# Three stages on one core: matmul order between heads, and attention and first layer in one block

## The chip, the cores and the metric

The kernel runs on one core of a Trainium2 chip. The metric is the time of one execution in microseconds (us); lower is better. The engines are named PE (TensorE, matmuls), ACT (ScalarE), DVE (VectorE), POOL (GpSimd) and SP (SyncE, which issues nearly all transfers here). Each engine runs its own list of instructions in order, and they wait for each other by semaphores.

## The reference

Three stages follow each other. Attention over 2 x 8 heads with 768 tokens of 64 numbers, masked by a hash: a score counts only where the signs of six projections of q and of k agree.

```python
mask = q_bucket[:, :, :, None] == k_bucket[:, :, None, :]
scores = np.where(mask, scale * (q @ k.T), -1e9)
scores -= max(scores); attn = exp(scores); attn /= sum(attn) + 1e-9
x = attn @ v                          # 1536 tokens x 512
h = np.maximum(x @ w_in, 0.0)         # first layer, 512 -> 2048
y = h * h @ w_out                     # 2048 -> 512
# experts: 8 experts of capacity 192, tokens assigned greedily by sorted logits y @ w_gate
out[mask_e] = np.maximum(y[mask_e] @ w1[e], 0.0) @ w2[e]
```

## The kernel before

**Attention (lines 74 to 681).** Sixteen heads are taken in the order of `ORDER`, in pairs: an even and an odd head. Pairs 1 to 6 run in a hardware loop on PE and on DVE; pair 0 and the last heads are written out. For a head n the parts are: `scores` (six steps of 128 queries, one matmul pass) from which DVE takes row maxima (`row_max`, `max_done`); `rows`, which turns the maxima and a sum of v into rows by small matmuls; ACT copies these rows (`qb`, line 317, `v_sum_hi`, line 318) and DVE makes `v_low`; `scores_t`, the transposed scores with the maximum folded in, six steps; ACT takes the exponential of each (`expo`, line 324, into `pt`); `fallback` and `weighted` multiply by v and accumulate in PSUM. Each `weighted` is one half of a step and shows as two records, as its operands are plain fp32. `scores` of head n+1 are mixed into head n on PE. There is one PSUM slot of two banks for the transposed scores, so `scores_t` j+1 waits for `expo` j.

During an even head the next pair is prepared: `t_k` and `t_q` transpose k and q, ACT copies the high parts (`k_high`, `q_high`, line 313), DVE subtracts for the low parts (`k_low`, `q_low`, line 391), `z_k` and `z_q` project them (lines 512 to 514), and DVE makes the bits (`k_bits`, `q_bits`). SP copies the parts from there into the operands of each head (`assemble`, lines 168 to 181): it first waits until all `scores_t` of the head two before are through, then issues eight copies; `q_high` of the next pair waits until those of the odd head have landed (lines 306 to 313).

When a head is through, DVE copies the numerator (line 426) and ACT the denominator (line 330); DVE takes reciprocals in four quarters (`invert`, line 432), POOL divides (`divide`, line 271), ACT and POOL split the quotient into `xt_hi` and `xt_lo` (`high`, line 335; `low`, line 277). The weights of the first layer are loaded by SP during the heads, in 17 transfers counted by `w_ready`.

**First layer (lines 706 to 1049).** A block of its own; a block ends when all engines have reached its end. Four chunks of 384 tokens by 16 tiles of 128 hidden units. For a tile g ACT makes `wi_hi` and `wo_hi` (lines 829, 836) and POOL `wi_lo` and `wo_lo` (lines 750, 756), in two buffers each. PE runs `hidden` (12 matmuls, line 965) into one of two banks, ACT relu and square (lines 842, 844), DVE the product `h` and the difference `h_lo` (lines 889, 892), and PE `rows` (9 matmuls, line 976) of the tile, one tile behind. The first chunk also finishes the last head: DVE takes reciprocals of two halves ahead of its tiles 0 and 1 (lines 907, 910), POOL divides after `both_low` of tile 0 (line 780), ACT and POOL split after tiles 2 and 3.

**Experts (lines 1052 to 1437).** Routing on DVE and PE in small steps, then eight experts, with gathers and scatters by POOL. DVE starts with a memset of the tail of `slot_onehot` (line 1331); POOL waits for the stores of y ahead of its first gather.

## Time and profile before

| | |
|---|---|
| median of 3 runs | 879.3 us (878.26 to 882.99) |
| the profiled execution's own time | 880.77 us |
| its span, first to last instruction | 879.0 us |
| mean granted TensorE clock | 0.961 |
| PE busy | 815.8 us, 93% |
| DVE, ACT, POOL busy | 411.1, 321.6, 281.6 us |

Attention takes the span up to 312.5 us, the first layer from there to about 610 us, routing and experts the rest. The page gives the span in 40 slices of 22 us. In a timeline each line is one or several like instructions in order of time; "idle" in brackets is how long the engine had nothing to run before it, and who released it. A PE record starts when its operands begin to be read, and records overlap: the distance between two starts is the pace.

### The profile page before, as it was taken

What the parts mean: (1) busy time and instruction counts of PE and PEld (TensorE: products, weight loads), DVE (VectorE), ACT (ScalarE), POOL (GpSimd) and SP (SyncE); (2) the same over time, 40 slices, a digit from 0 to 9 for tenths busy, and PEclk for the clock granted to TensorE, in tenths of its full rate; (3) what the DMA queues carried; (4) which work ended last, traced back from release to release, by engine and by line L of the source; (5) the groups of instructions that cost most, each with busy time, mean ns of one, the idle gap of its engine ahead of it and who ended that gap; (6) DMA issues with size and microseconds to landing.
All of it is one profiled execution on the core that took longest, in us unless ns stands there. A gap on an engine that the chain in (4) does not pass through costs nothing. (4 is left out here: it accounts for less than half of the span.)

```text
span 879.0 us, 13881 instructions
## 1 busy us (share of the span) xinstructions
PE 815.8 (93%) x4688; PEld 698.8 (79%) x4688; DVE 411.1 (47%) x884; ACT 321.6 (37%) x575; POOL 281.6 (32%) x283
## 2 busy tenths in 40 slices
PE   5999999999999969999999999997389998999996
PEld 3767777677776758999999999996279998999996
DVE  7466666666666545224223223423634554455410
ACT  1344434444344444554554555452011212112211
POOL 3022322223222246655665566562000101110101
PEclk8799999999999989999999999999579999999999
DMA  7345545567635300001000001000235453635351
GB/s 166 71 104 122 126 101 126 131 143 176 143 90 137 93 0 1 0 0 37 0 0 36 0 0 37 0 0 37 97 114 210 144 199 118 224 131 209 141 201 36
DMA packets 65763, 81.28 MB, mean 92 GB/s; under 512 B 41304, under 2 KB 41304, under 8 KB 65216
## 3 DMA queue, kind: packets, MB, share of 16 engines
q1 hardware_dynamic: 63680, 74.54, 30.8%
q0 software_dynamic: 2048, 6.29, 2.2%
q8 instruction: 20, 0.33, 0.1%
q14 instruction: 15, 0.12, 0.0%
HBM read 54.55 MB, written 6.29 MB: 69 GB/s over the span
## 5 line engine op out<-in xcount | busy, mean ns | idle before, releaser
L586 PE MATMUL banks<-pt,v_raw 128*128 128x384 f32 x384 | 149.3, 489 | 0.0
L324 ACT ACTIVATE pt<-banks 128x768 f32<-128x768 f32 x96 | 78.0, 812 | 137.5 <-PE banks L536 135.5
L889 DVE TENSOR_TENSOR h<-relu 128x384 f32<-128x384 f32 x64 | 42.1, 658 | 177.3 <-ACT relu L842 177.2
L750 POOL TENSOR_TENSOR wi_lo<-w_in_sb,wi_hi 128x512 fp32r<-128x512 f32 x64 | 84.0, 1313 | 95.3 <-ACT wi_hi L829 94.3
L403 DVE TENSOR_REDUCE mx<-banks 128x1 f32<-128x768 f32 x96 | 89.9, 951 | 30.3 <-PE banks L563 28.5
L1405 PE MATMUL banks<-x_cols,w_in_sb 128*128 128x192 f32 x512 | 96.1, 340 | 1.3 <-ACT x_cols L1189 1.1
L1419 PE MATMUL banks<-expert_hidden,w_out_sb 128*128 128x192 f32 x512 | 93.4, 333 | 0.0
L965 PE MATMUL banks<-xt_hi,wi_hi 128*128 128x384 f32 (+1 forms) x256 | 87.5, 342 | 6.2 <-POOL wi_lo L750 6.2
L756 POOL TENSOR_TENSOR wo_lo<-w_out_sb,wo_hi 128x512 fp32r<-128x512 f32 x64 | 83.8, 1309 | 15.0 <-ACT wo_hi L836 15.0
L1405 PEld LDWEIGHTS banks<-x_cols,w_in_sb 128*128 128x128 f32 x512 | 84.5, 195 | 3.7 <-issue 2.0
L965 PE MATMUL banks<-xt_lo,wi_hi 128*128 128x384 f32 (+1 forms) x256 | 87.0, 340 | 0.0
L965 PE MATMUL banks<-xt_hi,wi_lo 128*128 128x384 f32 (+1 forms) x256 | 86.8, 339 | 0.0
L1419 PEld LDWEIGHTS banks<-expert_hidden,w_out_sb 128*128 128x128 f32 x512 | 83.1, 192 | 0.8
L586 PEld LDWEIGHTS banks<-pt,v_raw 128*128 128x128 f32 x384 | 68.9, 189 | 15.3 <-issue 3.3
L535 PE MATMUL banks<-qa,ka 128*128 128x384 f32 x192 | 72.1, 376 | 8.0 <-ACT pt L324 4.7
L976 PE MATMUL banks<-wo_hi,h_hi 128*128 128x512 f32 x192 | 76.2, 397 | 2.2 <-DVE h_lo L892 2.1
L563 PE MATMUL banks<-kb,qb 128*128 128x384 f32 x192 | 74.5, 472 | 2.4 <-DVE qb L399 2.1
L976 PE MATMUL banks<-wo_hi,h_lo 128*128 128x512 f32 x192 | 76.3, 397 | 0.0
L976 PE MATMUL banks<-wo_lo,h_hi 128*128 128x512 f32 x192 | 76.0, 396 | 0.0
L536 PE MATMUL banks<-qb,kb 128*128 128x384 f32 x192 | 65.2, 339 | 0.0
L842 ACT ACTIVATE relu<-banks 128x384 f32<-128x384 f32 x64 | 31.5, 493 | 91.5 <-PE banks L965 91.5
L535 PEld LDWEIGHTS banks<-qa,ka 128*128 128x128 f32 x192 | 36.5, 190 | 29.3 <-ACT pt L324 15.1
(182 smaller groups left out, 1261.2 us busy)
## 6 DMA issues: line engine op xcount, KB each, us to landing
w_in_sb<-in_moe_w SPq DMA_DIRECT2D x8, 2048.0 KB, 9.5
w_out_sb<-in_moe_w SPq DMA_DIRECT2D x8, 2048.0 KB, 8.1
w_in_sb<-in_moe_w_in SPq DMA_DIRECT2D x8, 512.0 KB, 6.4
w_out_sb<-in_moe_w_out SPq DMA_DIRECT2D x8, 512.0 KB, 5.1
w_out_sb<-in_k SPq DMA_DIRECT2D x16, 192.0 KB, 3.6
w_out_sb<-in_q SPq DMA_DIRECT2D x16, 192.0 KB, 4.0
v_raw<-in_v SPq DMA_DIRECT2D x16, 192.0 KB, 3.7
kb<-k_hi SPq DMA_DIRECT2D x16, 192.0 KB
```

Source lines behind the costliest of these rows:

```text
L324: act.activation(halves(pt[j % 2]), both(ST), ACT.Exp, scale=SCALE).then_inc(ex, 1)
L403: dve.tensor_reduce(mx[:, j:j + 1], both((PREP, SM)[j % 2]), AX.XY, ALU.max).then_inc(mxs, 1)
L535: pe.matmul(ST[:, h, 0:HALF], ka[i][:, kc], qa[i][:, c], start=True, stop=False)
L536: last = pe.matmul(ST[:, h, 0:HALF], kb[i][:, kc], qb[i][:, c], start=False, stop=True)
L563: last = pe.matmul(slot[:, h, 0:HALF], qb[i][:, qcol], kb[i][:, h * HALF:(h + 1) * HALF], start=True, stop=True)
L586: last = pe.matmul(O[:, h, 0:HALF], v_raw[i][:, j, :], pt[j % 2][:, h * HALF:(h + 1) * HALF], start=False, stop=j == 5)
L750: pool.tensor_tensor(wil[i][:], wi[:].rearrange("p (k f) -> p k f", k=DT)[:, :, bass.ds(f * P, P)], wih[i][:].bitcast(fp32), ALU.subtract) ...
L756: pool.tensor_tensor(wol[i][:], wo[:, bass.ds(f * DM, DM)], woh[i][:].bitcast(fp32), ALU.subtract).then_inc(wols, 1)
L965: last = pe.matmul(PB[i][:, 0:HALF], w_[:, k, :], x_[:, xs], start=n == 0, stop=n == 3 * DT - 1)
L976: last = pe.matmul(PB[2 + t][:], h_[:, tc], w_[:], start=start and n == 0, stop=stop and n == 2, skip_group_check=True)
L1405: last = pe.matmul(PB[2 + f % 2][:, 0:CAP], w1s[i][:, k, f * P:(f + 1) * P], xgt[:, k, :], start=k == 0, stop=k == DT - 1)
L1419: last = pe.matmul(PB[4 + d % 2][:, 0:CAP], w2s[i][:, f, d * P:(d + 1) * P], hs[:, f, :], start=f == 0, stop=f == F2T - 1)
```

## The change

1. Order on PE. In an even head `t_k` now comes ahead of `scores_t` 1. All six `scores` of the next head come one `weighted` half earlier, and `rows` of the next head comes ahead of the last `weighted` half of the head's own fifth step instead of behind it. The same in odd heads for the last two `scores` pairs and `rows`.
2. Order on DVE in odd heads. All six row maxima and `max_done` come ahead of reciprocal quarters 2 and 3.
3. Attention and first layer are in one block. The split weights are allocated ahead of both, in a new function `weight_splits`. In the last head ACT makes the first three high parts between `expo` 2 and `expo` 3 (after a wait for all weights), and POOL the three low parts ahead of its last `divide`.
4. First chunk of the first layer. DVE takes four quarters of reciprocals, each behind a tile, instead of two halves ahead of tiles; POOL divides behind tile 5 instead of tile 0; the split of the quotient moves from tiles 2 and 3 to tiles 6 and 7. The counts of `relus` lose their head start of 2, and PE skips the waits for it at tiles 0 and 1.
5. Experts. The memset of `slot_onehot` moves from DVE to POOL, behind a wait for the stores, and PE waits for it (`padded`) ahead of its first list; DVE waits for the stores once ahead of its second level.

```diff
@@ attention: pool, act
+                if n == HEADS - 1:
+                    pool.drain()
+                    split["in_low"](pool, 0, 0, 0)
+                    split["in_low"](pool, 1, 1, 1)
+                    split["out_low"](pool, 0, 0, 0)
                 if i == 1:
                     divide(g)
...
+                if n == HEADS - 1:
+                    act.wait_ge(split["w_ready"], 16 * 17)
+                    split["in_high"](act, 0, 0)
+                    split["in_high"](act, 1, 1)
+                    split["out_high"](act, 0, 0)
                 expo(n, 3)
@@ attention: dve, odd
                 if nxt:
-                    row_max(n + 1, 0)
-                    row_max(n + 1, 1)
-                    row_max(n + 1, 2)
+                    for j in range(6):
+                        row_max(n + 1, j)
+                    max_done(n + 1)
                 invert(p, 2)
-                if nxt:
-                    row_max(n + 1, 3)
-                    row_max(n + 1, 4)
-                    row_max(n + 1, 5)
-                    max_done(n + 1)
                 invert(p, 3)
@@ attention: pe, even
-                scores_t(n, 0, p, 1)
                 if prepare:
                     t_k(p + 1)
+                scores_t(n, 0, p, 1)
                 fallback(n, 0)
...
                 weighted(n, 0, 1, 0)
+                scores(n + 1, 1, p, 0, nxt)
                 weighted(n, 0, 1, 1)
-                scores(n + 1, 1, p, 0, nxt)
+                scores(n + 1, 1, p, 1, nxt)
                 scores_t(n, 0, p, 3)
-                scores(n + 1, 1, p, 1, nxt)
+                scores(n + 1, 1, p, 2, nxt)
                 weighted(n, 0, 2, 0)
-                scores(n + 1, 1, p, 2, nxt)
+                scores(n + 1, 1, p, 3, nxt)
                 weighted(n, 0, 2, 1)
-                scores(n + 1, 1, p, 3, nxt)
+                scores(n + 1, 1, p, 4, nxt)
                 scores_t(n, 0, p, 4)
                 weighted(n, 0, 3, 0)
-                scores(n + 1, 1, p, 4, nxt)
+                scores(n + 1, 1, p, 5, nxt)
                 weighted(n, 0, 3, 1)
-                scores(n + 1, 1, p, 5, nxt)
                 scores_t(n, 0, p, 5)
                 weighted(n, 0, 4, 0)
+                rows(n + 1)
                 weighted(n, 0, 4, 1)
-                rows(n + 1)
@@ attention: pe, odd
                 scores_t(n, 1, p, 3)
+                if nxt:
+                    scores(n + 1, 0, p + 1, 2, None)
                 weighted(n, 1, 2, 0)
...
                 weighted(n, 1, 4, 0)
-                weighted(n, 1, 4, 1)
                 if nxt:
                     rows(n + 1)
+                weighted(n, 1, 4, 1)
@@ weight_splits
+    def in_high(act, f, i):
+        act.activation(wih[i][:], in_view(f), ACT.Copy).then_inc(wihs, 1)
...
+    def in_low(pool, g, f, i):
+        pool.wait_ge(wihs, g + 1)
+        pool.tensor_tensor(wil[i][:], in_view(f), wih[i][:].bitcast(fp32), ALU.subtract).then_inc(wils, 1)
@@ first_layer: pool
-            both_low(0, 2, 1, 0)
+            for g in range(6):
+                both_low(g, g + 2, g + 1, g % 2)
             pool.drain()
             pool.wait_ge(inverted, 1)
             pool.tensor_tensor(xo[top, :], num[top, :], rden[top, :], ALU.mult).then_inc(divided, 1)
@@ first_layer: dve
+                for j in range(4):
+                    hidden(c * FT + j, j % 2)
+                    if first:
+                        quarter = slice(j * S // INV, (j + 1) * S // INV)
+                        dve.reciprocal(rden[top, quarter], den[top, quarter])
@@ first_layer: pe
-                pe.wait_ge(relus, g + 1)
+                if past(g, 2):
+                    pe.wait_ge(relus, g - 1)
@@ experts: pool, dve, pe
+            pool.wait_ge(stored, 16 * CHUNKS)
+            pool.memset(oh[:, CAP:OHW], 0.0).then_inc(padded, 1)
...
+                    if l == 1 and not past(s, 1):
+                        dve.wait_ge(stored, 16 * CHUNKS)
...
-            dve.memset(oh[:, CAP:OHW], 0.0)
...
+                    if not past(s, 1):
+                        pe.wait_ge(padded, 1)
@@ build
+            split = weight_splits(nc, shared, sem, wi, wo, w_ready)
+            with nc.Block() as block:
+                attention(nc, block, sem, banks, ident, finish, xt_hi, xt_lo, wo, split, load_in, load_out, load_gate, q, k, v, proj)
+                K = routing_constants(nc, shared)
+                first_layer(nc, block, sem, PB, ident, K, finish, xt_hi, xt_lo, split, wg, L, stored, y_rows)
```

## Rows read from the trace of the kernel before

**Rows 1.** The page, the span in 40 slices: granted clock in tenths.

```profile
PEclk8799999999999989999999999999579999999999
```

**Rows 2.** Timeline of PE at the seam: start us, us, engine, line, operation.

```profile
309.76 2.74 PE L586 MATMUL banks<-pt,v_raw 128*128 128x384 f32 x8
318.67 0.69 PE L965 MATMUL banks<-xt_hi,wi_hi 128*128 128x384 f32 x1 [6.17 <-POOL wi_lo L750]
...
322.30 0.34 PE L965 MATMUL banks<-xt_hi,wi_hi 128*128 128x384 f32 x1
...
330.82 0.50 PE L976 MATMUL banks<-wo_hi,h_hi 128*128 128x512 f32 x1 [2.07 <-DVE h_lo L892]
...
338.74 0.34 PE L965 MATMUL banks<-xt_hi,wi_hi 128*128 128x384 f32 x1
```

**Rows 3.** Table of stretches, all engines: busy us, then PEclk, DMA share, GB/s.

```profile
332.00:333.00 1.00, 1.00 (x5) 0.76 (x4) 0.92 (x2) 0.00 (x0) 1.00 (x1) 0.53 0.00 0
```

**Rows 4.** Timeline of PE at a boundary into an odd head, loop pair.

```profile
191.16 0.52 PE L572 MATMUL banks<-identr,mn 128*3 128x128 f32 x6
...
191.92 0.91 PE L586 MATMUL banks<-pt,v_raw 128*128 128x384 f32 x2
192.88 0.44 PE L535 MATMUL banks<-qa,ka 128*128 128x384 f32 x1
```

**Rows 5.** Timeline of ACT at the same boundary.

```profile
192.03 0.80 ACT L317 ACTIVATE qb<-banks 3x768 fp32r<-3x768 f32 x1 [1.26 <-PE banks L573]
```

**Rows 6.** Timeline of DVE ahead of the same boundary.

```profile
188.26 1.95 DVE L403 TENSOR_REDUCE mx<-banks 128x1 f32<-128x768 f32 x2 [0.73 <-PE banks L563]
```

**Rows 7.** Timeline of PE at a boundary into an even head, loop pair.

```profile
169.80 1.45 PE L586 MATMUL banks<-pt,v_raw 128*128 128x384 f32 x4
...
173.10 0.43 PE L535 MATMUL banks<-qa,ka 128*128 128x384 f32 x1 [0.33 <-ACT qb L317]
...
174.95 0.44 PE L535 MATMUL banks<-qa,ka 128*128 128x384 f32 x1 [0.26 <-ACT pt L324]
```

**Rows 8.** Timeline of all engines in the same even head.

```profile
174.73 0.60 SPq L163 DMA_DIRECT2D qa<-q_lo  x1
...
178.67 0.81 ACT L313 ACTIVATE q_hi<-banks 128x768 fp32r<-128x768 f32 x1 [1.20 <-DMA qa<-q_lo]
...
179.52 0.96 DVE L391 TENSOR_TENSOR q_lo<-banks,q_hi 128x768 fp32r<-128x768 f32 x1 [1.06 <-ACT q_hi L313]
...
180.53 0.19 PEld L512 LDWEIGHTS banks<-q_hi,proj_hi 128*128 128x128 f32 x1 [0.22 <-DVE q_lo L391]
```

**Rows 9.** Timeline of all engines in head 0, the second transposed score.

```profile
27.11 0.69 PE L535 MATMUL banks<-qa,ka 128*128 128x384 f32 x1 [0.90 <-ACT pt L324]
```

**Rows 10.** Timeline of ACT, last head and start of the first layer.

```profile
305.98 0.81 ACT L324 ACTIVATE pt<-banks 128x768 f32<-128x768 f32 x1 [1.18 <-PE banks L536]
...
313.46 0.84 ACT L335 ACTIVATE xt_hi<-x_out 128x768 fp32r<-128x768 f32 x1
316.57 1.15 ACT L829 ACTIVATE wi_hi<-w_in_sb 128x512 fp32r<-128x512 f32 x2 [2.27 <-PEq L77]
```

**Rows 11.** Timeline of SP, its last issue of the attention.

```profile
289.30 0.47 SPq L1468 DMA_DIRECT2D w_gate_sb<-in_moe_w_gate  x1
```

**Rows 12.** Transfers from 285 to 312 us: count, KB each, median us to landing.

```profile
w_gate_sb<-in_moe_w_gate SPq DMA_DIRECT2D x1, 16.0 KB, 5.6
```

**Rows 13.** Timeline of all engines, POOL and DVE at the seam.

```profile
314.38 1.80 POOL L277 TENSOR_TENSOR xt_lo<-x_out,xt_hi 128x768 fp32r<-128x768 f32 x1 [6.74 <-ACT xt_hi L335]
...
323.08 0.56 DVE L889 TENSOR_TENSOR h<-relu 128x384 f32<-128x384 f32 x1 [4.01 <-ACT relu L842]
...
326.97 1.83 POOL L780 TENSOR_TENSOR x_out<-num,rden 64x768 f32<-64x768 f32 x1 [0.20 <-DVEq L911]
326.99 2.23 DVE L889 TENSOR_TENSOR h<-relu 128x384 f32<-128x384 f32 x1
```

**Rows 14.** Timeline of DVE at the start of the routing.

```profile
610.58 0.22 DVE L1331 MEMSET slot_onehot<- 128x192 uint32 x1 [0.39 <-PEq L712]
```

More of the change, by code:

```diff
@@ L71, in past, with attention @@
     return not (isinstance(m, int) and m < k)
-def attention(nc, banks, ident, finish, xt_hi, xt_lo, spare, load_in, load_out, load_gate, q, k, v, proj):
+def attention(nc, block, sem, banks, ident, finish, xt_hi, xt_lo, spare, split, load_in, load_out, load_gate, q, k, v, proj):
     with ExitStack() as ctx:
@@ L703, in routing_constants, with weight_splits, pair, in_view @@
         upto=sb("members_up_to_tile", [P, 2 * NT + 1], fp16))
-def first_layer(nc, PB, ident, K, finish, xt_hi, xt_lo, wi, wo, wg, L, w_ready, stored, y_rows):
+def weight_splits(nc, ctx, sem, wi, wo, w_ready):
+    def pair(name, shape):
+        return [ctx.enter_context(nc.sbuf_tensor(f"{name}{i}", shape, f32r)) for i in range(2)]
+    wih, wil, woh, wol = pair("wi_hi", [P, DT, P]), pair("wi_lo", [P, DT, P]), pair("wo_hi", [P, DM]), pair("wo_lo", [P, DM])
+    wihs, wils, wohs, wols = (sem("split_" + n) for n in ("wihs", "wils", "wohs", "wols"))
+    def in_view(f):
+        return wi[:].rearrange("p (k f) -> p k f", k=DT)[:, :, bass.ds(f * P, P)]
+    def out_view(f):
+        return wo[:, bass.ds(f * DM, DM)]
+    def in_high(act, f, i):
+        act.activation(wih[i][:], in_view(f), ACT.Copy).then_inc(wihs, 1)
+    def out_high(act, f, i):
+        act.activation(woh[i][:], out_view(f), ACT.Copy).then_inc(wohs, 1)
+    def in_low(pool, g, f, i):
+        pool.wait_ge(wihs, g + 1)
+        pool.tensor_tensor(wil[i][:], in_view(f), wih[i][:].bitcast(fp32), ALU.subtract).then_inc(wils, 1)
+    def out_low(pool, g, f, i):
+        pool.wait_ge(wohs, g + 1)
+        pool.tensor_tensor(wol[i][:], out_view(f), woh[i][:].bitcast(fp32), ALU.subtract).then_inc(wols, 1)
+    return dict(wih=wih, wil=wil, woh=woh, wol=wol, wihs=wihs, wils=wils, wohs=wohs, wols=wols, w_ready=w_ready,
+                in_high=in_high, out_high=out_high, in_low=in_low, out_low=out_low)
+def first_layer(nc, block, sem, PB, ident, K, finish, xt_hi, xt_lo, split, wg, L, stored, y_rows):
     with ExitStack() as ctx:
@@ L865, in chunk @@
                 if first:
-                    tile_high(2, 4, 3, 0)
-                    act.wait_ge(divided, 1)
-                    act.activation(xt_hi[top, last_pair], xo[top, :], ACT.Copy).then_inc(head_high, 1)
-                    tile_high(3, 5, 4, 1)
-                with act.Fori(2 if first else 1, FT // 2 - 1) as fp:
+                    for g in range(2, 8):
+                        tile_high(g, g + 2, g + 1, g % 2)
+                        if g == 6:
+                            act.wait_ge(divided, 1)
+                            act.activation(xt_hi[top, last_pair], xo[top, :], ACT.Copy).then_inc(head_high, 1)
+                with act.Fori(4 if first else 1, FT // 2 - 1) as fp:
                     for i in range(2):
@@ L953, in _ @@
         def _(pe):
-            pe.wait_ge(w_ready, 16 * 17)
+            pe.wait_ge(split["w_ready"], 16 * 17)
             pe.sem_inc(rows_done, 2)
@@ L1145, in gather @@
                 pool.wait_ge(list_ready, s + 1)
-                if not past(s, 1):
-                    pool.wait_ge(stored, 16 * CHUNKS)
                 if past(s, 2):
@@ L1444, in build, with sem @@
         PB = [banks[i // 2][:, i % 2] for i in range(8)]
[L1445 to L1446 removed]
+        def sem(name):
+            return ctx.enter_context(nc.semaphore(name))
+        w_ready, stored = sem("w_ready"), sem("stored")
         ident = ctx.enter_context(nc.sbuf_tensor("ident", [P, P], fp32))
```

103 lines of the change are left out of this document (30 added, 73 removed).

## The prediction

> **What bounds the kernel now.** I read the page's slices first: TensorE's (PE's) granted clock is full except in three places, the start, one slice near 330 us and the one from 615 us [rows 1]. The timeline of PE then shows why at the second place: from its last attention records, which end at 312.50, to 318.67 it is idle for 6.17 us, and it stops again ahead of 330.82 [rows 2]; the table of stretches has the clock at 0.53 just after 332 [rows 3]. That is the seam between attention and the first layer. Last I read the timeline of each engine at a head boundary. In the middle of a head PE's records follow each other without idle time; at a boundary there are gaps. So PE's own order bounds the attention, and what it waits for is a chain between engines at each boundary. Two sizes for what follows: eight records of weighted values, four halves, take 2.57 us (309.76 to 312.33, where the next could start), so a half is 0.64 us [rows 2]; a short record of 384 columns takes 0.174 us (twelve from 318.67 on excepted, which ran at half clock), so a transposed score step of four is 0.70.
>
> **Boundary into an odd head (8 of them).** Before: `rows` starts at 191.16 and the first transposed score of the next head at 192.88, 1.72 us later. ACT copies the row at 192.03 for 0.80 us, ending at 192.83, so ACT sets that start [rows 4, 5]. Counted with the weighted half that stood ahead of `rows` it is 0.64 + 1.72 = 2.36 us. After the change this half follows `rows`: 0.76 us for `rows` (191.16 to 191.92), 0.64 and 0.64 is 2.04 us, more than ACT's 1.67 us. Gain 0.32 us; and since PE no longer restarts from a stop, its four score records take 0.70 us instead of some 0.81 (the first record alone 0.44 instead of 0.34), gain 0.11 [rows 4]. The exponential, denominator and fallback behind it are an unchanged ACT chain and all start that much earlier.
> Is DVE ready? All score steps move ahead by one weighted half, as `rows` does. Today's last maxima end at 190.21, and `max_done` lasts until `rows` at 191.16, 0.95 us [rows 4, 6]. Walking the new order from the second projection (180.53): scores 0 end at 182.68, 1 at 183.66, 2 at 184.70, 3 at 185.69, 4 at 186.68, 5 at 188.37; a maximum takes 0.96 us and starts 0.21 us behind its scores, so the last ends at 189.55 and `rows` can start at 190.50, against 190.34 at which PE is ready. That stop of 0.15 us stands in place of today's 0.13. I keep 0.45 us for a boundary, 8 x 0.45 = **3.6 us**. With the reciprocal no longer between the maxima of an odd head PE loses 0.1 us less there, 7 heads, **0.7 us**.
>
> **Boundary into an even head.** PE's own side promises more: 0.3 to 0.6 us at the row copy, and the transposes of k fill the 1.85 us between the two first score steps (173.10 to 174.95) [rows 7]. But the next limit is near. SyncE starts the eight copies for the odd head when the last transposed scores are through, at 169.80 [rows 7]; the last, `q_lo`, is issued at 174.73, and ACT's `q_hi`, which overwrites its source, waits for it until 178.67 [rows 8]. Then come 0.81 us of ACT and, from 179.52, 0.96 of DVE, and the second projection starts at 180.53, with PE's weight load released by `q_lo` [rows 8]. So this projection stands 10.73 us behind the last transposed scores today, and no instruction of that chain moves. PE's new path to it: 0.79 to `rows`, 2.13 to the next head, 1.34 for two stages ahead of the transposes, 0.57 for these, 0.70, then fallback (held by ACT's denominator until 2.79 after the head began), 0.35, 0.65, 1.28, 1.05, 0.70: 0.79 + 2.13 + 2.79 + 4.03 = 9.7 us. PE arrives 1.0 us early and waits. I count **0 us** for the six boundaries in the loop (reciprocals two and three after `max_done` add 1.3 us to the chain of `rec`, which ends 1.6 us before ACT's denominator asks for it). Bounds: 0 to 0.75 us each, that is up to 4.5 us. The boundary 13 to 14 prepares no pair: **0.35 us**.
>
> **Head 0.** Between its first two transposed scores PE idles 0.90 us at half clock [rows 9]; the transposes of pair 1 now fill this. They have what they need (no wait for their data is seen), so 1.1 us go, and an earlier rise of the clock could make it 1.6. I take **1.1 us**, bounds 0.6 to 1.6.
>
> **Last head.** ACT gets three copies between its third and fourth exponential. Two such took 1.15 us together at 316.57, so three take some 1.7 [rows 10]. The weights have landed long before: the last transfer of the queue is issued at 289.30 and lands 5.6 us later, at 294.9 [rows 11, 12], and ACT asks for them at 304.8 in the old time; only a landing 10 us late would cost anything. ACT is idle 1.18 us ahead of an exponential [rows 10] and PE has some 0.2 us of slack, so PE stops for about 0.3 us (bounds 0 and 0.9: all of it hidden, or the 1.7 us less only half of ACT's idle time and slack): **-0.3 us**. POOL's three differences (1.3 us each) then run ahead of its divide; nobody needs that divide until ACT's `high(7)`, over 2 us later.
>
> **The seam.** Before: PE is free at 312.33 and the fifth hidden tile starts at 338.74 [rows 2]: 26.4 us. Four hidden tiles of 2.08 us (twelve records of 0.174) and three row groups of 2.08 are 14.6 us of it. The rest, 11.8 us, is the idle start (6.35), half clock behind it (1.6), the stop at 330.82 (2.24 with the restart) and half clock again (1.7) [rows 2, 3]. All of this goes except what comes in its place.
> The Trainium skill ("TensorE: Matmul & The Clock Gate", Back-to-back issue gap) has N/2.4 + 2.5 ns for one warm matmul; that would give an estimate of 13.6 us for those 14.6. The rows are slower, and I use the rows.
> What is late next: hidden 0 starts at once (its first halves are split), ends 2.1 us after attention, and hidden 1 covers 2.08 us more. Then row group 0 needs `h_lo` 0. ACT runs the denominator and `high(7)` first and is free in time for relu 0; before, `h` started 0.78 us behind the last record of hidden 0 (322.30 to 323.08), so it now starts 2.08 + 0.78 = 2.86 us behind attention [rows 2, 13]. At this moment POOL is in `low(7)`, which starts when `high(7)` ends (+2.05) and lasts 1.80 [rows 10, 13]. DVE's product of two SBUF tiles took 0.56 us at 323.08, beside no POOL work, and 2.23 us at 326.99 when POOL had started its 1.83 us product at 326.97: it ends 0.42 us behind POOL [rows 13]. So `h` ends at +4.28, then `h_lo` meets POOL's next difference (1.3 us) in the same way and ends at +5.95; row group 0 starts at +6.0, where PE is ready at +4.16. A stop of 1.85 us. By the Trainium skill ("SBUF — State Buffer", Who interferes with whom) VectorE with two SBUF inputs and a GpSimd read exclude each other for the whole instruction; the trace agrees, by the 2.23 us. Later groups have 4.1 us of PE work between a hidden tile and its row group, and the reciprocal quarters (1.3 us each) and POOL's divide, now after the sixth tile, fit. Gain: 11.8 - 1.85 = **9.9 us**.
>
> **Routing.** DVE's memset leaves the head of its chain [rows 14], 0.14 us from start to start of it and the next instruction. The new waits for `stored` and `padded` come 3 and 20 us after what they wait for: **0.1 us**. Only a store landing 4 us later than now would cost anything.
>
> **Sum.** 3.6 + 0.7 + 0.35 + 1.1 - 0.3 + 9.9 + 0.1 = 15.4 us. The profiled execution took 880.77 us (span 879.0, 1.8 around it); the median of the runs is 879.3. The same 15.4 off the median gives **863.9 us**, 865.4 for an execution like the profiled one.
>
> **Rivals.** (a) *The clock falls after the new stop.* The stop of 2.07 us at 330.82 was followed by half clock from about 332, the one of 6.17 as well [rows 2, 3]; the stop of 1.85 us is a little shorter. Price 1.7 us: 865.6. (b) *No lock stop.* If `h` gets in ahead of POOL, row group 0 is on time: 1.85 us less, 862.1. (c) *The transfer chain gives way*: if the `q_lo` landing moves forward with PE, the six even boundaries give up to 0.75 us each: 859.4. Against it: ACT waits for that landing, and the eight issues take SyncE 4.9 us from 169.80 on, whatever PE does behind it. (d) *The change doesn't do what it says at the seam*: PE still waits there for the weight copies, as if ACT reached them only after the head. Then some 4 us of the idle time stay, and part of the half clock: 869. Against it: ACT reaches them 7 us before the end. (e) *Slower than before.* The new waits of PE at each even boundary (0.3 ahead of the first projection, 0.6 ahead of the second) fall close together with the one at fallback; if the granted clock fell behind them, each of the 7 even heads would run some 3.4 us at half clock, 1.7 us, and odd boundaries the same: 15 x 1.7 = 25 us against 15.4, 889. It decides from 9 such falls on. Against it: today PE stops 0.6 and 0.4 us within 2 us at each boundary, and the clock in those slices, the third to the fourteenth, is 9 tenths or more [rows 1].
>
> **How the numbers follow.** Forecast 863.9: 45%. (a) 865.6: 18%. (b) 862.1: 15%. (c) 859.4: 12%. (d) 869: 7%. (e) 889: 3%. The range goes from 859.4 less half of a us for (c) up to 868, the forecast with (a) and the poor ends of head 0 and of the last head added: 859 to 868 leaves out (d), (e) and a part of (c) at its ends. A measurement of this kernel can tell about 0.5% (4.4 us) from no change. All cases but (e) lie more than 9 us below the median; allowing for two terms failing together, faster 0.95, same 0.02, slower 0.03.
>
> **What would show it.** Period of two heads in the loop 35.9 us instead of 36.45; the second projection still 10.7 us behind the last transposed scores, with PE waiting for DVE ahead of it; the row copy no longer in PE's waits into odd heads; no gap between attention and hidden 0, clock unbroken there; one stop near 2 us ahead of row group 0, released by DVE's `h_lo`, with `h` and `h_lo` near 1.4 us each beside POOL's `low(7)`; hidden tile 4 some 16.7 us behind the end of attention. I am wrong if the even boundaries gain (c), or if the loss moved to a place not walked here.

## The result, and the profile after

The changed kernel takes 874.11 us (median; 869.25 to 874.39), the kernel before on the same chip 881.03 us (878.26 to 882.99). The ratio is 0.9912, with a 95% interval of 0.9883 to 0.9942. It is faster beyond its interval, by 6.9 us (under 1%) where 15.4 were forecast; 863.9 us was predicted, with a range of 859 to 868, and the time lies above this range. The profiled execution took 874.02 us (span 872.3) against 880.77 us, so 6.75 us less, with the same granted clock of 0.961.

From the page of the changed kernel, busy time of PE and its granted clock in 40 slices:

```profile
PE 816.2 (94%) x4688; PEld 703.0 (81%) x4688; DVE 416.4 (48%) x885; ACT 321.6 (37%) x575; POOL 283.4 (32%) x284
...
PEclk8899999999999999999999999996589999999999
```

The slower slice at the seam, 8 tenths before (308 to 330 us), is gone, as forecast [rows 1]. The slow stretch behind the first layer now begins one slice earlier: 6 tenths from 589 us on, where the slice from 593 us had 9 before. So the mean clock is the same although the lower clock at the seam is gone (0.85 from 310 to 345 us before, 1.00 after): as much has come back elsewhere. Where the time went shows best in a table of the same moments in both profiled executions, read from the timelines of PE. In the first line, "before" is the end of its last eight records (309.76 plus 2.29, the time that the same eight take after the change).

| moment | before | after | gain | forecast |
|---|---|---|---|---|
| attention through | 312.05 | 308.87 | 3.2 | 5.45 |
| hidden tile 4 starts | 338.74 | 325.67 | 13.1 | 15.3 |
| last two row groups start | 598.96 | 588.07 | 10.9 | 15.3 |
| first matmul of the routing's counts | 613.92 | 605.17 | 8.75 | 15.3 |
| first transpose of an expert | 640.43 | 632.24 | 8.2 | 15.4 |
| end of the span | 879.0 | 872.3 | 6.7 | 15.4 |

So there are three losses: 2.3 us in the attention, 2.2 us in the first layer behind tile 4, and 4.2 us from there to the end. The seam itself brought 9.9 us, as forecast. Half of the shortfall, the 4.2 us, lies where the granted clock differs between executions, and most of it isn't settled by any run.

**The seam.** PE's timeline of the changed kernel (start us, us, engine, line, operation; in brackets the idle time and its releaser), answering [rows 2]:

```profile
303.79 0.45 PE L535 MATMUL banks<-qa,ka 128*128 128x384 f32 x1
...
306.58 2.74 PE L586 MATMUL banks<-pt,v_raw 128*128 128x384 f32 x8
308.87 0.63 PE L962 MATMUL banks<-xt_hi,wi_hi 128*128 128x384 f32 x1
...
315.08 0.51 PE L973 MATMUL banks<-wo_hi,h_hi 128*128 128x512 f32 x1 [1.59 <-DVE h_lo L890]
...
325.67 0.34 PE L962 MATMUL banks<-xt_hi,wi_hi 128*128 128x384 f32 x1
```

The first hidden tile follows the last weighted halves without a gap, where PE was idle for 6.17 us. One stop is left, 1.59 us ahead of row group 0, and the releaser is `h_lo`. The timeline of all engines shows why, answering [rows 13]:

```profile
311.22 1.86 POOL L272 TENSOR_TENSOR xt_lo<-x_out,xt_hi 128x768 fp32r<-128x768 f32 x1 [3.18 <-ACT xt_hi L335]
...
312.03 1.45 DVE L887 TENSOR_TENSOR h<-relu 128x384 f32<-128x384 f32 x1 [1.71 <-ACT relu L842]
...
313.57 1.46 DVE L890 TENSOR_TENSOR h_lo<-h,h_hi 128x384 fp32r<-128x384 f32 x1
```

`h` starts in the middle of POOL's `low(7)` and ends 0.40 us behind it; `h_lo` meets POOL's next difference. Both take 1.45 us in place of 0.56. Tile 4 starts 16.8 us behind the attention (forecast 16.7).

**A boundary into an odd head.** Timeline of all engines, answering [rows 4, 6]:

```profile
187.16 0.17 DVE L414 TENSOR_SCALAR has<-mx 128x6 f32<-128x6 f32 x1
...
187.41 0.17 DVE L416 SCALAR_TENSOR_TENSOR mn<-mx,has 128x6 fp32r<-128x6 f32 x1
...
187.46 0.73 POOL L245 MEMSET qb<- 1x768 f32 x1 [6.32 <-PE banks L536]
187.50 0.73 DVE L417 TENSOR_SCALAR mn<-has 128x12 fp32r<-128x12 f32 x1
188.31 0.33 PEld L572 LDWEIGHTS banks<-identr,mn 128*3 128x3 f32 x6 [0.88 <-DVEq L419]
188.31 0.52 PE L572 MATMUL banks<-identr,mn 128*3 128x128 f32 x6 [0.26 <-DVEq L419]
```

The last small instruction of `max_done` takes 0.73 us, for twelve elements a partition. In each even head it takes 0.17, and at the boundary into the last head too, where no memset is made. It starts just behind a memset of POOL, which clears a row of `qb`, and it ends when this memset has ended. PE waits for it ahead of `rows`. In the kernel before, the same memset met another instruction at this place:

```profile
189.98 0.73 POOL L250 MEMSET qb<- 1x768 f32 x1 [5.86 <-PE banks L536]
190.31 0.42 DVE L409 TENSOR_SCALAR has<-mx 128x6 f32<-128x6 f32 x1
190.82 0.17 DVE L411 SCALAR_TENSOR_TENSOR mn<-mx,has 128x6 fp32r<-128x6 f32 x1
190.91 0.17 DVE L412 TENSOR_SCALAR mn<-has 128x12 fp32r<-128x12 f32 x1
```

There it cost 0.25 us (0.42 in place of 0.17). I had read the whole 0.95 us of `max_done` as its length, and not looked at what stood beside it. Before, the memset began 0.33 us ahead of the first of the three instructions; the change moves them ahead by 3.15 us and the memset by 2.52, so it begins behind the first, 0.04 us ahead of the third, which then waits for nearly all of it.

**A boundary into an even head.** PE's timeline from the last transposed scores to the second projection, answering [rows 7, 8]:

```profile
167.38 0.81 PE L586 MATMUL banks<-pt,v_raw 128*128 128x384 f32 x2
...
170.88 0.81 PE L586 MATMUL banks<-pt,v_raw 128*128 128x384 f32 x2
171.53 0.82 PE L494 MATMUL banks<-ident,w_out_sb 128*128 128x128 f32 x6
...
178.04 0.44 PE L512 MATMUL banks<-q_hi,proj_hi 128*128 128x384 f32 x1 [0.37 <-DVE q_lo L396]
```

10.66 us lie from the end of the last transposed scores (where the first of these records starts) to the projection (10.73 before), and PE waits for `q_lo`: the chain of transfers holds, and the transposes of k now fill the wait that they were meant to fill, without a gain.

### The profile page after: what moved, and what is told of

It is laid out like the page before. It is cut to its first block and busy times, and to the rows that moved or that the text cites. A ratio compares the mean times of both kernels' runs of the same rounds, so it can differ in the third digit from the quotient of the medians.

```text
span 872.3 us, 13757 instructions
## 1 busy us (share of the span) xinstructions
PE 816.2 (94%) x4688; PEld 703.0 (81%) x4688; DVE 416.4 (48%) x885; ACT 321.6 (37%) x575; POOL 283.4 (32%) x284
## 5 line engine op out<-in xcount | busy, mean ns | idle before, releaser
L408 DVE TENSOR_REDUCE mx<-banks 128x1 f32<-128x768 f32 x96 | 91.7, 957 | 26.2 <-PE banks L563 23.3
L732 POOL TENSOR_TENSOR wo_lo<-w_out_sb,wo_hi 128x512 fp32r<-128x512 f32 x64 | 84.7, 1323 | 15.1 <-ACT wo_hi L724 15.1
L535 PE MATMUL banks<-qa,ka 128*128 128x384 f32 x192 | 78.3, 408 | 3.2 <-ACT pt L324 2.3
L1154 POOL DMA_INDIRECT out<-expert_out,token_list x16 | 15.0, 935 | 135.5 <-ACT expert_out L1195 133.1
```

The lines of the kernel that those rows point to most:

```text
L408: dve.tensor_reduce(mx[:, j:j + 1], both((PREP, SM)[j % 2]), AX.XY, ALU.max).then_inc(mxs, 1)
L535: pe.matmul(ST[:, h, 0:HALF], ka[i][:, kc], qa[i][:, c], start=True, stop=False)
L732: pool.tensor_tensor(wol[i][:], out_view(f), woh[i][:].bitcast(fp32), ALU.subtract).then_inc(wols, 1)
```

## Experiments

Each kernel ran beside the kernel before on the same chip. The ratio with its interval comes from all timed runs and can differ a little from the quotient of the medians. Where one execution is looked at, its timeline is used for the mechanism and not its time. One reading needs care: the first heads of two executions can start up to 0.9 us apart (first transposed scores of head 0), and a moment later in the attention holds this too.

### 1. The two halves of the change

`e1_order_only` is the kernel before with parts 1 and 2 of the change (the orders on PE and DVE). `e2_merge_only` is the changed kernel with the old orders.

> The kernel before with only the new order of PE and of DVE in the attention; blocks, weight splits, first layer and experts as before. Theory A (the head boundaries gave 3.2 of the 5.75 us forecast for them, since DVE's max_done meets POOL's memset of the free row at every boundary into an odd head): attention ends 3.4 to 3.6 us earlier than before (before: 312.3), the small operation of max_done that meets the memset takes 0.7 us instead of 0.17, two heads take 36.3 us. Rival B (the shortfall comes from the merged block or from the copies in the last head, not from the order): attention ends 5 us or more earlier here and two heads take 35.9 us. The seam is as before (PE idle 6 us, 26.4 us to hidden tile 4) by both.

> The changed kernel with the old order of PE and DVE in the attention: only one block, early splits, reciprocal quarters and the moved memset. Theory A: attention ends within 0.5 us of before (0.3 us later for the three copies), hidden tile 4 starts 16.5 us behind attention's end, the pace of a tile in the first layer is 4.19 us as in the changed kernel (before 4.165), so that 1.8 us of the 9.9 us of the seam are given back there. Rival B (the slower tile pace is chance or comes from the order): pace 4.165. Time against before: -7 to -8 us by A, -10 us by B.

Measured: the orders alone 876.29 us against 879.29, ratio 0.9983 (0.9946 to 1.0020). The merge alone 873.32, ratio 0.9939 (0.9911 to 0.9967). The interval of the orders alone holds 1, so its gain is read from the profile and not shown by the time; the profiled execution (882.98 us) has two pieces at the lower clock in the experts, of 6.8 and 3.4 us. In this profile the order alone brings the first hidden matmul from 318.67 to 315.45, so 3.2 us, as much as in the changed kernel (there 0.3 us for ACT's copies is already taken off). The small operation beside the memset takes 0.72 us and two heads 36.4 us, as theory A has them. With the merge alone the first record of hidden tile 5 comes 9.6 us earlier (342.90 to 333.29), and the pace of a tile in the first layer is 4.203 us; with the orders alone it stays 4.173. What follows: the 9.9 us of the seam are the merge's, and the orders bring about 3 us, not 5.75. The order's loss is its own, and not one of the two together.

### 2. The memset of the free row

```diff
@@ attention: pool, ahead of the memset of qb's first row
+                pool.wait_ge(mns, n + 2)
```

The memset now waits until `max_done` of the next head is through; it is the changed kernel otherwise.

> The changed kernel; POOL's memset of the free row of qb waits until DVE has finished max_done of that boundary. Theory A (that memset and DVE's small operations block each other): all three operations of max_done take 0.17 us, the wait of PE's rows into odd heads for DVE (0.26 us) goes, two heads take 36.0 us instead of 36.3, attention ends 2 to 3 us earlier than in the changed kernel (at about 306.5 instead of 309.1). Rival B (DVE's maxima are late for another reason): rows into odd heads still start 10.27 us behind the second projection, and the attention's end stays within 0.5 us.

Measured: 867.86 us, ratio 0.9872 (0.9837 to 0.9908). Timeline of all engines at the boundary of above:

```profile
186.50 0.17 DVE L418 TENSOR_SCALAR mn<-has 128x12 fp32r<-128x12 f32 x1
186.74 0.28 PEld L573 LDWEIGHTS banks<-identr,mn 128*3 128x3 f32 x3 [0.32 <-DVEq L420]
186.75 0.47 PE L573 MATMUL banks<-identr,mn 128*3 128x128 f32 x3
186.81 0.73 POOL L246 MEMSET qb<- 1x768 f32 x1 [6.68 <-DVEq L420]
```

`mn` takes 0.17 us, PE doesn't stop ahead of `rows`, and the period of two heads falls from 36.38 to 35.91 us (35.9 was forecast for the change). The first hidden matmul comes at 306.54, 2.3 us earlier than in the changed kernel. This equals the shortfall of the attention, but in part by chance: this execution began head 0 0.9 us later than the changed kernel's, so from there on it gained 3.2 us. The size of the conflict is read best over one boundary, from the last record of the even head's transposed scores to the fourth of the next head's. At the last one, where neither kernel makes a memset, the two records are, before and after:

```profile
295.31 0.33 PE L536 MATMUL banks<-qb,kb 128*128 128x384 f32 x1
...
299.13 0.34 PE L536 MATMUL banks<-qb,kb 128*128 128x384 f32 x1
```

```profile
292.17 0.33 PE L536 MATMUL banks<-qb,kb 128*128 128x384 f32 x1
...
295.67 0.34 PE L536 MATMUL banks<-qb,kb 128*128 128x384 f32 x1
```

| us between the two records | before | changed | memset later |
|---|---|---|---|
| seven boundaries with a memset | 3.94 | 3.92 | 3.50 |
| the boundary into the last head | 3.82 | 3.50 | 3.50 |

So the new order gains 0.32 us where no memset is near, the conflict costs PE 0.12 us before and 0.42 after, and the seven boundaries gain 0.02 us each. The edit takes away both, what the change added (0.30) and what the kernel before already paid (0.12). No run of the changed kernel stood on the chip of this experiment and the next, so their times are compared with the kernel before alone.

### 3. The stop at the seam

```diff
@@ pool: low(7) leaves attention, into the first layer's first chunk
             for g in range(6):
                 both_low(g, g + 2, g + 1, g % 2)
+                if g == 2:
+                    split["last_low"](pool)
```

> The changed kernel; POOL's difference xt_lo of the last pair moves from ahead of the first layer to behind the tiles' sixth low part (after both_low of tile 2). Theory A (it holds the port against DVE's h and h_lo of tile 0): h and h_lo of tile 0 take 0.56 us each instead of 1.45, the stop of PE ahead of row group 0 (1.59 us) goes, and hidden tile 4 starts 14.6 to 15.0 us behind attention's end instead of 16.5. Rival B (the stop is ACT's or the reciprocals'): stop stays over 1 us.

Measured: 868.83 us, ratio 0.9899 (0.9864 to 0.9935). Timeline of all engines, then of PE:

```profile
312.63 0.56 DVE L889 TENSOR_TENSOR h<-relu 128x384 f32<-128x384 f32 x1 [1.71 <-ACT relu L844]
...
313.27 0.56 DVE L892 TENSOR_TENSOR h_lo<-h,h_hi 128x384 fp32r<-128x384 f32 x1
```

```profile
313.76 0.34 PE L964 MATMUL banks<-xt_hi,wi_lo 128*128 128x384 f32 x1
313.93 0.46 PE L975 MATMUL banks<-wo_hi,h_hi 128*128 128x512 f32 x1
```

With POOL elsewhere both instructions take 0.56 us and row group 0 follows without a stop; tile 5 starts 19.74 us behind the first hidden matmul in place of 21.00, so the stop had cost 1.3 us net (tile 4 comes 1.5 us earlier, and 0.25 us of it go again where `low(7)` now lies). The mechanism written down for it holds.

### 4. The chain of transfers

The two copies of bits, which have nothing to do with `q_high`, go last among SyncE's eight, with semaphores of their own, so that `k_high` and `q_high` no longer wait for them.

```diff
@@ assemble
-                sp.dma_start(kb[i][FEATURES, :].bitcast(fp32), kbit[bits(i), :]).then_inc(kb_in[i], 16)
...
-                sp.dma_start(qb[i][FEATURES, :].bitcast(fp32), qbit[bits(i), :]).then_inc(qb_in[i], 16)
...
+                sp.dma_start(kb[i][FEATURES, :].bitcast(fp32), kbit[bits(i), :]).then_inc(kbit_in[i], 16)
+                sp.dma_start(qb[i][FEATURES, :].bitcast(fp32), qbit[bits(i), :]).then_inc(qbit_in[i], 16)
```

> The changed kernel; of the copies that SP makes for a head the two small ones with the bits go last, with semaphores of their own, so that k_high and q_high of the next pair wait for the six large ones alone. q_lo is issued 1.6 us earlier behind the last transposed scores. Theory A (the transfer chain holds the second projection in place at 10.66 us behind the last transposed scores): the second projection moves to 9.7 to 10.0 us, PE's wait there for q_lo (0.4 us a time, 2.5 in all) goes, attention ends 3 to 5 us earlier than in the changed kernel. Rival B (ACT or DVE holds it): stays at 10.6, attention ends within 0.5 us.

Measured: 866.68 us, ratio 0.9836 (0.9771 to 0.9901). PE's timeline:

```profile
166.43 0.81 PE L599 MATMUL banks<-pt,v_raw 128*128 128x384 f32 x2
...
176.55 0.42 PE L521 MATMUL banks<-q_hi,proj_hi 128*128 128x384 f32 x1
```

The projection comes 10.12 us behind the last transposed scores (9.7 to 10.0 expected) and nothing stops PE there. The period falls to 35.78 us, with the memset's conflict still in place. So it was this chain that held the even boundaries, and the price of it is some 0.6 us for a pair of heads. The attention ends 2.1 us earlier than in the changed kernel, less than the 3 to 5 expected; some 0.4 us of the gap is a later start of head 0.

### 5. All three

`e7_all_three` is the changed kernel with the edits of 2, 3 and 4, and `e12_three_again` the same kernel on another chip. `e8_changed_again` is the changed kernel, on the chip of the first.

> The changed kernel with the three edits of e3, e4 and e5 together. If the three causes are separate: attention ends 6 to 8 us earlier than in the changed kernel, the stop ahead of row group 0 is gone (1.6 us more), time 8 to 9 us below the changed kernel's. If the gains of e3 and e5 are the same time counted twice: 4 to 6 us below.

> The changed kernel once more, five rounds, for the granted clock of each run. Theory A (some 1.5 to 3 us of the shortfall are half clock at the end of the first layer and in the experts, which falls differently from run to run): runs differ by 3 us or more, and the faster ones have the higher mean clock; about 2 us of time for 0.003 of clock. Rival B: runs agree within 1 us.

> The kernel with the three corrections once more, on the same chip as the one with the pad. Both theories: 4.203 us a tile, attention's end and the first hidden matmul as in its first run (305.9), and about 0.984 of before; what of its time differs from the first run goes with the granted clock.

Measured: 864.92 us, ratio 0.9846 (0.9775 to 0.9918), and 865.44 us, ratio 0.9833 (0.9803 to 0.9862). The changed kernel beside the first: 869.55 us, ratio 0.9878 (0.9826 to 0.9929); its runs span 8 us, the slowest with the lowest clock, as theory A has it. The three together are faster than the kernel before; against the changed one the medians differ by 4.6 us, with intervals that overlap, so that the times alone don't show it. 8 to 9 us were expected if the three causes are separate, 4 to 6 if two of them share their time: it is the second. Hidden tile 5 starts at 325.62, 4.25 us earlier than in the changed kernel (329.87). The gains don't add up: alone, the memset's edit brings 2.3 us at that point, the transfers' 2.1, and the stop 1.3, together 5.7. The later starts of head 0 (0.4 to 0.9 us) don't change this. The period is 35.75 us with the memset and the chain both mended, against 35.91 and 35.78 with one of them. Each pair of heads then has its even half (`rows` to `rows`) 19.2 us long, 1.2 less than in the changed kernel, and its odd half 16.5, 0.6 more. In the odd half a wait of 0.26 us for an exponential is left, and one of 0.18 us whose releaser the trace doesn't name. What holds the odd half wasn't tested.

### 6. The pace of the first layer

In the changed kernel a tile takes 4.203 us (ten row groups from the 50th to the 60th), before 4.173. The instructions are the same. First guess: the order of the split tiles in SBUF decides. `e6_split_address` allocates `wo_hi`, `wo_lo`, `wi_hi`, `wi_lo` in this order.

> The changed kernel; the four pairs of split weight tiles are allocated in another order (wo_hi, wo_lo, wi_hi, wi_lo instead of wi_hi, wi_lo, wo_hi, wo_lo), nothing else. Theory A (the slower pace of row groups, 0.240 us instead of 0.227 to 0.233 behind each record of h_hi with wo_hi, hangs on where the split tiles lie): the pace of a tile changes from 4.19 us by 0.02 or more, either way. Rival B (it is another cause): 4.19 again.

Measured: 870.28 us, ratio 0.9886 (0.9821 to 0.9952), pace 4.203: the guess fell. The pace doesn't come from the order of the matmuls either, as experiment 1 shows (4.173 with the orders alone, 4.203 with the merge alone). Then the whole placement was moved in the kernel before: its split tiles are allocated ahead of the routing constants, as in the change, instead of behind them. For this its experts are those of the changed kernel (the memset of `slot_onehot` on POOL with its waits).

```diff
@@ build of the kernel before, ahead of the routing constants
+            splits = [[shared.enter_context(nc.sbuf_tensor(f"{name}{i}", shape, f32r)) for i in range(2)]
+                      for name, shape in (("wi_hi", [P, DT, P]), ("wi_lo", [P, DT, P]), ("wo_hi", [P, DM]), ("wo_lo", [P, DM]))]
```

> The kernel before, with two blocks and its old order, and only the place of the split tiles changed: they are allocated ahead of the routing constants, as in the changed kernel (with the changed kernel's experts function, since slot_onehot then lies over y_rows_sb and its memset has to wait for the last store). Theory A (the slower tile pace of every kernel with the merged block, 4.203 us instead of 4.173, comes from where the tiles lie in SBUF): the pace in the first layer is 4.20 here too. Rival B (it comes from the merged program, or from the waits for relu that lost their head start): the pace stays 4.173. Attention's end and the seam are as before by both, 312.3 and 26.4 us.

Measured: 884.6 us against 880.42, ratio 1.0054 (1.0013 to 1.0095), pace 4.203. PE's timeline, one whole tile each, of this kernel, of the changed one and of the one before:

```profile
450.43 0.34 PE L962 MATMUL banks<-xt_hi,wi_hi 128*128 x1
...
454.63 0.34 PE L962 MATMUL banks<-xt_hi,wi_hi 128*128 x1
```

```profile
450.01 0.39 PE L973 MATMUL banks<-wo_hi,h_hi 128*128 128x512 f32 x1
...
454.21 0.47 PE L973 MATMUL banks<-wo_hi,h_hi 128*128 128x512 f32 x1
```

```profile
451.45 0.34 PE L965 MATMUL banks<-xt_hi,wi_hi 128*128 x1
...
455.62 0.34 PE L965 MATMUL banks<-xt_hi,wi_hi 128*128 x1
```

4.20, 4.20 and 4.17 us. So the slower pace comes with the place of the tiles: a kernel with the old order and the old blocks, in whose first layer nothing else differs, has it too. Over 64 tiles the pace makes 1.9 of the 4.2 us between the medians; this kernel also has the changed experts, and the rest wasn't looked for. Then I tried to find what of the place it is. In the kernel before the split tiles start 18,720 bytes a partition higher, the size of the routing constants. `e10_three_and_pad` adds an unused tile of 2336 bytes ahead of them to the kernel with three edits, `e11_pad_32` one of 32 bytes to the changed kernel, and `e13_pad_both` and `e14_pad_behind` one of 5856 bytes ahead of `h` in the kernel with three edits, with and without the first pad.

> The kernel with the three corrections, and an unused tile of 2336 bytes a partition ahead of the split tiles, which gives these the place that they have in the kernel before, taken modulo 8 KB. Nothing that is executed changes. Theory A (the first layer's pace hangs on where the split tiles lie within such a stretch): 4.173 us a tile in place of 4.203, so 1.9 us less over 64 tiles than the kernel with three corrections, ratio to before near 0.982. Theory B (it hangs on their absolute place, or on where they lie against the other tiles): 4.203 us a tile, and the same time as without the pad.

> The changed kernel with an unused tile of 32 bytes a partition ahead of the split tiles. Theory A1 (the pace hangs on how the tiles lie to a 64-byte line alone): 4.173 us a tile. Theory B (on something coarser): 4.203 us a tile as in the changed kernel.

> The kernel with the three corrections, with unused tiles of 2336 bytes ahead of the split tiles and of 5856 bytes between the routing constants and the tiles of the first layer (h, relu and their parts). Both groups then lie where they lie in the kernel before, taken modulo 8 KB; with the first pad alone only the split tiles did. Theory A2 (the pace hangs on where both groups lie to each other and to the unmoved tiles, modulo 8 KB): 4.173 us a tile. Theory B (on the absolute place, or on a larger stretch): 4.196 to 4.203.

> The kernel with the three corrections, with the unused tile of 5856 bytes ahead of the first layer's own tiles alone. These then lie to the split tiles as in the kernel before modulo 8 KB (24 KB apart instead of adjoining), while the split tiles lie to the unmoved tiles as in the changed kernel. Theory A3 (the pace hangs on how these two groups lie to each other): 4.173 us a tile. Theory A2 (both have to be in place) or B: about 4.20.

Measured: paces of 4.196, 4.196, 4.202 and 4.206 us. The kernel with the pad took 865.82 us, ratio 0.9856 (0.9817 to 0.9894), beside 865.44 without it; the other three ran once each (875.97, 874.39 and 870.23 us), for their pace alone.
## Why the prediction was right or wrong

**Head 0 and the boundary behind it** (1.1 + 0.45 forecast): at head 1 the gain is 1.54 us beyond an earlier start of 0.52 that the execution had. The sum is right by luck: head 0 alone gained 1.53, near the upper bound that was written for an earlier rise of the clock (it rises at 29.4 us instead of 31.7), and the boundary behind it gained 0.02. In the second profile of the changed kernel head 0 gained 1.10.

**Boundaries into odd heads** (8 x 0.45 forecast): this is the step that failed. Seven of them gained 0.02 us each, and the last one 0.32. In the loop, a pair of heads gained 0.11 to 0.15 us in place of 0.55, 0.7 us over six pairs in place of 3.3. My walk put the end of `max_done` 0.95 us behind the last maxima, as it was before, and found a stop of 0.15 us ahead of `rows` in place of 0.13. But those 0.95 us held a conflict whose size hangs on when the memset falls. After the change the last maxima end as I had walked, and the memset meets a later one of the three small instructions, early in its own run: 0.56 us where there had been 0.25. PE's stop is 0.26 us, `rows` starts 10.27 us behind the second projection (178.04 to 188.31) where the walk gives 9.97, and PE's weighted records restart behind `rows` with another 0.1. Experiment 2 shows it: of the 0.43 us that each of the seven boundaries fell short, 0.30 is what the conflict costs more than before, and 0.13 is the walk's own, as the last boundary has it too (0.32 in place of 0.45) without any memset. That the period without the conflict comes to 35.91, the forecast, is therefore in part luck: the edit also takes away the 0.12 us that the kernel before paid. Over seven boundaries the step cost 3.0 us. Head 0's 0.4 us and the earlier start of 0.5 stand on the other side, and so the attention's end is 2.3 us short. The 0.1 us for the reciprocal came to 0.07 a head.

The Trainium skill ("SBUF — State Buffer", Who interferes with whom) lists `tensor_scalar` among the instructions of VectorE that can take both port pairs, and then VectorE or GpSimd blocks for the whole instruction of the other, whichever comes second. The rows agree: the two `tensor_scalar` that began beside the memset, one in each kernel, lasted to its end (0.73 and 0.42 us), and the `scalar_tensor_tensor` ahead of the changed kernel's, which began 0.05 us ahead of the memset, kept its 0.17. I had used the same section for `h` at the seam and not for a memset; it would have pointed to this one.

**Boundaries into even heads** (0): right, with the waits of PE where they were expected, and experiment 4 shows the chain as the cause. Rival (c) fell.

**Last head** (-0.3): right. ACT's timeline has the copies behind the third exponential:

```profile
300.54 0.81 ACT L324 ACTIVATE pt<-banks 128x768 f32<-128x768 f32 x1 [1.81 <-PE banks L536]
301.37 1.16 ACT L721 ACTIVATE wi_hi<-w_in_sb 128x512 fp32r<-128x512 f32 x2
302.43 0.61 ACT L724 ACTIVATE wo_hi<-w_out_sb 128x512 fp32r<-128x512 f32 x1
302.95 0.79 ACT L324 ACTIVATE pt<-banks 128x768 f32<-128x768 f32 x1
```

The attention's end lost 0.28 us against the heads ahead of it.

**The seam** (9.9): right in size, in the place of the one stop and in its cause. The profile gives the stop as 1.59 us where 1.85 was written. Rivals (a), (b) and (d) fell, and so did (e), as the slices of the attention have 9 tenths or more: the clock stays at its full level behind the stop (1.00 in the stretches from 312 to 342 us), `h` did meet POOL, and the weight copies were early.

**Behind the seam** (0 forecast, -2.2 measured up to the last two row groups). The gain is 13.1 us at tile 4, 12.5 at tile 11 and 10.9 at the last two. The first 0.6 us is mostly POOL's work for the last head's quotient, the division behind tile 5 and the split at tiles 6 and 7, where four row groups follow each other in 4.28 to 4.60 us: I had walked that it fits, and it doesn't quite. `h` beside the division takes 2.20 us, its `h_lo` then meets POOL's next difference, and PE stops for 0.25 us; some of POOL's differences have 1.60 us instead of 1.29. The other 1.6 us is the pace, 0.03 us a tile. I had no term for where tiles lie, and no row of the kernel before would have given one.

**From the last two row groups to the end** (+0.1 forecast, -4.2 measured). Here the granted clock differs. Tables of stretches of 5 us, counted from the last two row groups (busy us of PE, PEld, DVE, ACT and POOL, then granted clock, DMA share and GB/s), before and after; the last row is one in the experts, after:

```profile
603.96:608.96 5.00, 3.44 (x29) 3.16 (x29) 1.98 (x3) 1.06 (x3) 0.00 (x0) 1.00 0.42 157
608.96:613.96 5.00, 1.05 (x9) 0.96 (x10) 3.09 (x13) 0.00 (x0) 0.00 (x0) 0.80 0.00 0
```

```profile
593.07:598.07 5.00, 3.49 (x22) 3.29 (x22) 1.29 (x2) 1.01 (x3) 0.00 (x0) 0.79 0.42 157
598.07:603.07 5.00, 3.30 (x17) 3.21 (x16) 1.81 (x8) 0.00 (x0) 0.42 (x1) 0.50 0.00 0
...
692.00:702.00 10.00, 7.98 (x50) 7.51 (x51) 1.11 (x4) 1.53 (x4) 0.00 (x0) 0.66 0.59 215
```

Before, the clock falls to its lower level, 1.2 GHz, some 13 us behind the start of the last two row groups (0.80 is two fifths of the second stretch); after, it falls some 8 us behind it, and PE's last matmuls of the first layer (3.30 us busy where the same stretch before has 1.05) run at that level. That is 2.1 us. And in the experts there is a piece of 6.8 us at the lower level from 695 us on, with a loss of 1.5 us; the kernel before shows none in this execution. Is this the change's doing? The stretch from the last two row groups to the routing's first counts takes 15.0 us before and 17.1 after. With the same code from there on it takes 14.8 (`e2`, `e4`, `e6`, `e11`), 15.1 to 15.4 (`e3`, `e7`, `e12`), 16.6 to 16.7 (`e14`, and the changed kernel again) and 17.1 to 17.7 (`e5`, `e9`, `e10`, `e13`), and with the code of before 16.6 (`e1`). So either code has both values. In the 11 timed runs of the kernel before beside `e8` the time went from 876.33 us at a clock of 0.960 to 889.28 at 0.955, a spread of 13 us, wider than the whole gain, and the changed kernel's six from 868.73 (0.967) to 876.68 (0.958). The piece in the experts doesn't belong to the kernel: the second profile of the changed one has its own from 723 us on, 10.2 us long, and of the two profiles with three edits one has none and the other 3.4 us near 750. I read these 3.6 us as the clock's and not the change's. For the 2.1 us that is argued and not shown, as each kernel has one or two profiles, and the two of a kernel agreed (17.1 and 16.7, 15.3 and 15.1); part 5 of the change was never run by itself, and this part stays open. The last 0.6 us, in the routing's small steps, is no chance. From the first counts to the first transpose of an expert it takes 26.5 us in both profiles with the experts of before, and 26.9 to 27.2 in all thirteen with one block and the new experts (26.7 with two blocks, `e9`). In the changed kernel's rows 0.1 us of it is DVE's new wait for the stores, 0.3 us an idle time of DVE ahead of its fourth `reaches` for which the trace names no wait, and 0.1 us PE's wait for the gathered rows. So the term of the routing, +0.1, had the wrong sign as well; what makes DVE idle is open.

**The sum by what was measured:** 15.4 forecast, less 2.3 (3.0 at seven boundaries, mostly the conflict, less the luck of the start and of head 0), 0.6 (the last head's quotient), 1.6 (places of tiles) and 4.2 (3.6 the clock's by the argument above, 0.6 the routing's) is 6.7 us. With the failed step right the time would have been near 871 us, still above the range. With the changed kernel beside the three edits, on another chip, the median stood 10.2 us below that of before; the two measurements' intervals overlap (0.9883 to 0.9942, and 0.9826 to 0.9929). The range should have had room for the clock on its upper side: the runs of before had shown 4.7 us between them, and I gave no term for it. Its upper end doesn't follow from its terms either: 863.9 + 1.7 + 0.5 + 0.6 is 866.7, and 868 was written.

## What to carry to other kernels

A short instruction's duration in the trace may hold a wait for another engine's: before a chain is moved, compare each of its links with the same link elsewhere in the kernel (0.42 against 0.17 us here), and walk where the neighbour falls after the move, too. When a seam between stages goes, walk the next chunk of both engines that share ports; that was worth the effort here, as 9.9 us were forecast and 9.9 came. A boundary that lacks the neighbour, like the last one here, tells what the conflict costs without a new run. And a forecast for a kernel whose clock falls in places should carry the spread of its own runs in its range.

## What the runs showed of the hardware that was not expected

- A memset on POOL of one partition by 768 elements (0.73 us) blocks `tensor_scalar` instructions of DVE of six or twelve elements a partition until it ends: 0.73 and 0.42 us in place of 0.17.
- The place of tiles in SBUF changes the pace of the same matmuls by 0.7%: 4.173 or 4.203 us a tile, with values between (4.196) for pads of 32 and of 2336 bytes.
- A stop of 1.59 us ahead of row group 0 left the granted clock at 1.00; before, a stop of 2.07 us was followed by 0.53 [rows 2, 3].
